# Convolution and two MLPs on one core: the taps' band by another way through DRAM, the first steps reordered

## The chip, the cores and the metric

The kernel runs on one core of one Trainium2 chip. Its time is the device time of one execution in microseconds, here the median of several runs. The engines are TensorE (PE, its weight loads shown as PEld), VectorE (DVE), ScalarE (ACT), GpSimd (POOL) and SyncE (SP), which here issues all DMAs, in program order. Each engine works through its own queue in order and waits on semaphores.

## What is computed

```python
# x: (2, 4096, 192), weight: (8 heads, 7 taps); 24 channels per head
w = weight - np.max(weight, axis=-1, keepdims=True)
w = np.exp(w)
w = w / (np.sum(w, axis=-1, keepdims=True) + 1e-09)
out = np.einsum('hk,bskhg->bshg', w, x_unf)   # causal convolution over 7 positions
...
h = x @ w_in1                                  # first MLP, 192 -> 2048 -> 192
x = np.maximum(0.01 * h, h) @ w_out1
...
h = x @ w_in2                                  # second MLP
P = a[0] + a[1] * h + a[2] * h2 + a[3] * h3
Q = 1.0 + np.abs(b[0]) * np.abs(h) + np.abs(b[1]) * h2
out = (P / (Q + 1e-06)) @ w_out2
```

## The kernel before

The 8192 tokens go through in 16 blocks of 512 (`COLS`). A block is convolved on TensorE (`convolve`, L673): per head, a 110 x 104 matrix of taps (`band`, each row the taps' row moved by one) is the weight, and five tiles of 104 tokens with 6 tokens of halo stream past. ScalarE and VectorE copy the result out of PSUM (`copy_conv`), TensorE transposes it (`transpose_x`, L687, L688), and ScalarE and VectorE split it (`split_xt`) into a high part and a low part, so that fp32r products keep fp32's accuracy. `xs[0]` holds three parts: high and low of the first 128 channels, and the stacked high and low of the last 64. The first MLP's input to the second is split the same way into `xs[1]` (`split_x2`).

The MLPs run in pairs of hidden tiles: 8 pairs per block (`STEPS`), 128 in all. For pair m, `up` (L713) makes ten passes, five for each half: parts 0, 0, 1, 2, 2 of `xs`. Then come the leaky ReLU, its high part and its low part (L447, L451, L601), and `down` (L723 to L733), ten passes. For the second MLP, the steps between `up` and `down` are |h|, the slope and the first power on ScalarE (L390, L398, L405), the denominator on POOL (L337), the reciprocal (L411, L414), and polynomial, quotient, product and residue on VectorE (L593, L595, L575, L581, L587). The second MLP's pair n runs in step n together with the first MLP's pair n + 10 (`LEAD`), so the steps begin at -10. A step's place in its block is its phase, n modulo 8. In phase 7 a block is convolved, in phase 6 transposed, in phase 7 the second MLP's input is split.

The order on each engine is written out by hand, in `step(n)` of that engine. TensorE does `up` of the second MLP, then convolution, transposes or output transposes if the phase has them, then `up` and `down` of the first MLP. Block 0 is convolved in front of step -10 and block 1 in step -4. Block 2 is convolved in step -1. Before the first convolution TensorE runs `WARM_UP` matmuls on the identity, once POOL has made it.

The start also loads the weights. The weights of both MLPs come in 16 pieces (`order`), staged in seven buffers (`stage_weights` on SP), and each is split into a high part on ScalarE (`split_hi`, L373) and a low part on VectorE (`split_lo`, L510 or L515 and L517). How many pieces are split behind each pair is the tuple `share` in `split_with`. A piece of `w_in` takes one operation on each engine; a piece of `w_out` one on ScalarE and two on VectorE.

The band is made thus: SP loads `weight` to all 128 partitions; VectorE and ScalarE make the softmax; POOL has zeroed two rows of 852 numbers on one partition (L328), into which VectorE writes the taps (L545); SP writes both rows to DRAM (L301), and reads them back to 110 partitions, each shifted by one element (L303), as 110 x 8 pieces of 104 numbers. `band` is laid out by head, so that the weight of head h, `band[:, h, :]`, is contiguous in each partition.

Of the kernel before, what the change touches and what calls it, by code (L numbers as in the profile page):

```python
# [27 lines left out]
P = 128  # L28
# [14 lines left out]
WARM_UP = 30  # L43


def conv_mlp_mlp(nc: bass.Bass, x, weight, w_in1, w_out1, w_in2, w_out2, a, b, out):
# [24 lines left out]
    with ExitStack() as ctx:  # L71
# [31 lines left out]
        band = sb("band", [CROWS, H, CT])  # L103
        taps = sb("taps", [P, H, K])
        tap_stat = sb("tap_stat", [P, 3, H])
# [3 lines left out]
        conv_row = conv_sb[:, :, :].rearrange("p a c -> p (a c)")  # L109
        out_row = out_cm[:, :, :].rearrange("p a c -> p (a c)")  # L110

        tap_rows = [t[0:1, 0:HEADS * ROW].rearrange("p (h j) -> p h j", h=HEADS) for t in (conv_row, out_row)]
        tap_dram = nc.dram_tensor("tap_rows", (H, ROW), F32, kind="Internal").ap()
# [30 lines left out]
        s_const = sem("consts_loaded")  # L144
# [5 lines left out]
        s_row = sem("tap_row_steps")  # L150
# [110 lines left out]
        def _(sp):  # L261
# [27 lines left out]
            sp.dma_start(taps[:, :, :], weight.partition_broadcast(P)).then_inc(s_const, 16)  # L289
            sp.dma_start(coef_a[:, :], a.partition_broadcast(P)).then_inc(s_const, 16)  # L290
            sp.dma_start(coef_b[:, :], b.partition_broadcast(P)).then_inc(s_const, 16)
            sp.wait_ge(s_zero, 1)
            load_x(0)

            stage_weights(0)
            stage_weights(1)
            sp.wait_ge(s_row, 4)
            for half, row in enumerate(tap_rows):  # L300
                sp.dma_start(tap_dram[half * HEADS:(half + 1) * HEADS, :], row).then_inc(s_row_out, 16)  # L301
            sp.wait_ge(s_row_out, 32)
            sp.dma_start(band[:, :, :], bass.AP(tap_dram.tensor, 0, [[1, CROWS], [ROW, H], [1, CT]])).then_inc(s_band, 16)  # L303
# [20 lines left out]
        def _(pool):  # L324
            nc.gpsimd.memset(zero_halo[:, :], 0.0).then_inc(s_zero, 1)
            nc.gpsimd.memset(eye[:, :], 0.0).then_inc(s_eye, 1)
            for row in tap_rows:
                nc.gpsimd.memset(row, 0.0).then_inc(s_row, 1)  # L328
# [32 lines left out]
        def _(act):  # L361
# [64 lines left out]
            def step(n):  # L426
# [11 lines left out]
                if n >= 0 and phase != CONV_AT:  # L438
                    slope(n)
                if runs(conv_block(n), BLOCKS):  # L440
                    copy_conv(conv_block(n))
                if n >= 0:
                    first_power(n)
                    if phase == CONV_AT:
                        slope(n)
# [54 lines left out]
        def _(dve):  # L500
# [25 lines left out]
            dve.wait_ge(s_const, 48)  # L526
            stat = [tap_stat[:, k, :] for k in range(3)]

            def over_taps(v):
                return v.unsqueeze(2).to_broadcast([P, H, K])  # L530
# [11 lines left out]
            dve.wait_ge(s_row, 2)  # L542
            for half, row in enumerate(tap_rows):
                heads = slice(half * HEADS, (half + 1) * HEADS)
                V.tensor_tensor(row[:, :, CT - 1:CT - 1 + K], taps[0:1, heads, :],  # L545
                                tap_stat[0:1, 2, heads].unsqueeze(2).to_broadcast([1, HEADS, K]),
                                ALU.mult).then_inc(s_row, 1)

            V.scalar_tensor_tensor(coef_b[:, :], coef_b[:, :], -1.0, coef_b[:, :],
                                   ALU.mult, ALU.max).then_inc(s_coef, 1)  # L550
# [105 lines left out]
            split_lo(0)  # L656
            split_lo(1)
            copy_conv(0)
# [3 lines left out]
            V.tensor_tensor(eye2[:, :], eye[:, 0:DR], eye[:, DR:P], ALU.add).then_inc(s_eye2, 1)  # L662
            every_step(step, tail)

        @block.tensor
        def _(pe):
            T = nc.tensor

            def convolve(c):

                pe.wait_ge(s_x, 16 * (CTILES + 1) * (c + 1))
                for h in range(H):
                    last = T.matmul(conv_ps(c, h // HEADS)[:, h % HEADS], band[:, h, :],  # L673
# [30 lines left out]
            def up(m, pair0, dst, rest_ready, done):  # L704

                for half in range(2):
# [3 lines left out]
                    for j, (lhs, part) in enumerate(terms):  # L710
                        if half == 0 and j == 3:
                            rest_ready()
# [23 lines left out]
            def step(n):  # L736
# [15 lines left out]
                if runs(n, PAIRS):  # L752
                    if phase == 0:
                        pe.wait_ge(s_x2_lo, 2 * (n // STEPS) + 1)
                    if n == 0:
                        pe.wait_ge(s_wlo, 2 * PIECES)
# [4 lines left out]
                    def x2_rest_ready():  # L761
                        if phase == 0:
                            pe.wait_ge(s_x2_lo, 2 * (n // STEPS) + 2)

                    up(1, n, hidden_2(n), x2_rest_ready, s_h2)


                if convolves:
# [25 lines left out]
                def up_1():  # L794
                    if runs(m0, PAIRS):
                        if m0 in (0, STEPS // 2):
                            pe.wait_ge(s_wlo, 2 if m0 == 0 else 5)
                        if transposes:
                            pe.wait_ge(s_xt_lo, 2 * (m0 // STEPS) + 1)

                        if convolves and conv_block(n) > 1:
                            pe.wait_ge(s_conv_a, conv_block(n) + 1)
                            pe.wait_ge(s_conv_b, conv_block(n) - 1)
                        if leaves:
# [3 lines left out]
                        def xt_rest_ready():  # L808
                            if transposes:
                                pe.wait_ge(s_xt_lo, 2 * (m0 // STEPS) + 2)  # L810

# [102 lines left out]
```

## Time and profile before

| | us |
|---|---|
| median of 3 runs | 1302.13 |
| lowest and highest | 1301.85, 1303.23 |
| the profiled execution | 1303.33 |
| its span, first to last instruction | 1300.7 |
| TensorE busy in the span | 1254.8 |
| VectorE, ScalarE, POOL busy | 1039.7, 1042.9, 611.3 |
| mean granted clock of TensorE | 0.987 |

Times in the trace count from the first instruction. The profiled execution is 2.6 us longer than its own span, which leaves out what lies around the program. A group of matmuls such as "x16" counts passes: an fp32 matmul is two passes, so the eight of a convolution are 16. The clock is given as a share of full speed, 2.4 GHz.

### The profile page before, as it was taken

What the parts mean: (1) busy time and instruction counts of PE and PEld (TensorE: products, weight loads), DVE (VectorE), ACT (ScalarE), POOL (GpSimd) and SP (SyncE); (2) the same over time, 40 slices, a digit from 0 to 9 for tenths busy, and PEclk for the clock granted to TensorE, in tenths of its full rate; (3) what the DMA queues carried; (4) which work ended last, traced back from release to release, by engine and by line L of the source; (5) the groups of instructions that cost most, each with busy time, mean ns of one, the idle gap of its engine ahead of it and who ended that gap; (6) DMA issues with size and microseconds to landing.
All of it is one profiled execution on the core that took longest, in us unless ns stands there. A gap on an engine that the chain in (4) does not pass through costs nothing.

```text
span 1300.7 us, 14911 instructions
## 1 busy us (share of the span) xinstructions
PE 1254.8 (96%) x5788; PEld 1034.8 (80%) x5788; DVE 1039.7 (80%) x901; ACT 1042.9 (80%) x1025; POOL 611.3 (47%) x264
## 2 busy tenths in 40 slices
PE   6979999999999999999999999999999999999866
PEld 5768888888888888888888888888888888878744
DVE  2648878888788888888888788878878788887886
ACT  3768888888888888888888888888888888888874
POOL 0014454545545455454454544545545445454563
PEclk8999999999999999999999999999999999999898
DMA  6300000000000000000000000000000000000000
GB/s 184 94 14 1 1 26 2 26 1 1 26 1 26 1 19 7 2 26 1 26 1 1 26 1 26 1 27 1 1 26 1 26 1 13 1 1 14 0 13 12
DMA packets 25092, 21.73 MB, mean 17 GB/s; under 512 B 2909, under 2 KB 23997, under 8 KB 25023
## 3 DMA queue, kind: packets, MB, share of 16 engines
q1 hardware_dynamic: 25023, 20.80, 5.5%
q8 instruction: 45, 0.74, 0.2%
q14 instruction: 24, 0.20, 0.0%
HBM read 14.49 MB, written 6.30 MB: 16 GB/s over the span
## 4 chain that ended last, share of the span: by engine, by line
PE 90%; POOL 3%; issue 3%; DVE 2%; ACT 2%; DMA 1%; POOLq 0%; SPq 0%; ACTq 0%; DVEq 0%
PE h L713 43%; PE acc L723 8%; PE acc L732 8%; PE acc L733 8%; PE acc L725 8%; PE acc L724 8%; PE h L673 2%; POOL lo L342 1%; POOL den L337 1%; PE h L700 1%; POOL pol L337 1%; PE h L699 1%; PE h L687 0%; PE h L688 0%; ACT hi L451 0%
## 5 line engine op out<-in xcount | busy, mean ns | idle before, releaser
L713 PE MATMUL h<-xs,wa 128*128 128x512 f32 x2530 | 608.8, 392 | 16.4 <-DVE den L587 4.8
L337 POOL TENSOR_TENSOR den<-den,rec 128x1024 f32<-128x1024 f32 x125 | 300.9, 2407 | 665.7 <-DVE den L587 415.5
L713 PEld LDWEIGHTS h<-xs,wa 128*128 128x128 f32 x2530 | 475.6, 189 | 124.5 <-issue 9.2
L342 POOL TENSOR_TENSOR lo<-den,rec 128x1024 fp32r<-128x1024 f32 x124 | 299.4, 2414 | 6.7 <-DVE den L587 6.7
L575 DVE SCALAR_TENSOR_TENSOR hi<-pol,coef_a,rec 128x1024 fp32r<-128x1024 f32 x118 | 151.6, 1285 | 109.8 <-issue 68.8
L732 PE MATMUL acc<-lo,wb 128*128 128x512 f32 x512 | 201.1, 393 | 8.5 <-POOL lo L342 8.5
L723 PE MATMUL acc<-hi,wb 128*128 128x512 f32 x512 | 204.7, 400 | 2.7 <-ACT out_cm L464 1.4
L390 ACT ACTIVATE rec<-h 128x1024 f32<-128x1024 f32 x125 | 128.4, 1027 | 97.4 <-PE h L713 90.6
L725 PE MATMUL acc<-hi,wb 128*128 128x512 f32 x512 | 200.8, 392 | 0.0
L724 PE MATMUL acc<-hi,wb 128*128 128x512 f32 x512 | 200.7, 392 | 0.0
L733 PE MATMUL acc<-lo,wb 128*128 128x512 f32 x512 | 200.4, 391 | 0.0
L593 DVE TENSOR_TENSOR pol<-pol,h 128x1024 f32<-128x1024 f32 x125 | 152.6, 1220 | 58.8 <-ACT pol L405 55.5
L601 DVE TENSOR_TENSOR lo<-h,hi 128x1024 fp32r<-128x1024 f32 x128 | 156.2, 1220 | 46.5 <-ACT hi L451 46.5
L447 ACT ACTIVATE h<-h 128x1024 f32<-128x1024 f32 x128 | 129.3, 1010 | 61.8 <-PE h L713 61.8
L411 ACT ACTIVATE rec<-den,one 128x1024 f32<-128x1024 f32 x125 | 143.8, 1150 | 35.1 <-POOL den L337 35.1
L398 ACT ACTIVATE den<-rec,coef_b 128x1024 f32<-128x1024 f32 x125 | 155.9, 1247 | 3.1
L581 DVE SCALAR_TENSOR_TENSOR den<-den,hi 128x1024 f32<-128x1024 f32 x125 | 154.2, 1234 | 4.3
L587 DVE SCALAR_TENSOR_TENSOR den<-pol,coef_a,den 128x1024 f32<-128x1024 f32 x118 | 151.6, 1285 | 4.1
L595 DVE SCALAR_TENSOR_TENSOR pol<-pol,coef_a,h 128x1024 f32<-128x1024 f32 x118 | 151.2, 1281 | 4.2
L405 ACT ACTIVATE pol<-h,coef_a 128x1024 f32<-128x1024 f32 x125 | 149.4, 1195 | 0.4
L414 ACT ACTIVATE rec<-rec 128x1024 f32<-128x1024 f32 x128 | 135.9, 1062 | 4.1
L451 ACT ACTIVATE hi<-h 128x1024 fp32r<-128x1024 f32 x128 | 131.6, 1028 | 8.5 <-PE acc L733 4.6
(105 smaller groups left out, 959.4 us busy)
## 6 DMA issues: line engine op xcount, KB each, us to landing
out<-out_tok SPq DMA_DIRECT2D x16, 384.0 KB, 2.8
x_tok<-in_x SPq DMA_DIRECT2D x64, 82.5 KB
rec<-in_moe_w_out SPq DMA_DIRECT2D x4, 384.0 KB, 4.4
x_tok<-in_x SPq DMA_DIRECT2D x16, 78.0 KB
pol<-in_moe_w_out SPq DMA_DIRECT2D x3, 384.0 KB, 4.0
pol<-in_moe_w_in SPq DMA_DIRECT2D x2, 512.0 KB, 6.2
den<-in_moe_w_in SPq DMA_DIRECT2D x2, 512.0 KB, 4.7
rec<-in_moe_w_in SPq DMA_DIRECT2D x4, 256.0 KB, 5.4
```

What stands on the lines that cost most here:

```text
L337: nc.gpsimd.tensor_tensor(den_of(n)[:, :], den_of(n)[:, :], rec[n % RECS][:, :], ALU.mult).then_inc(s_den, 1)
L342: nc.gpsimd.tensor_tensor(lo2[n % 2][:, :], den_of(n)[:, :], rec[n % RECS][:, :], ALU.mult).then_inc(s_lo2, 1)
L398: nc.scalar.activation(den_of(n)[:, :], rec[n % RECS][:, :], ACT.Identity, scale=coef_b[:, 1:2], bias=coef_b[:, 0:1]).then_inc(s_slope, 1)
L581: V.scalar_tensor_tensor(den_of(n)[:, :], den_of(n)[:, :], 1.000001, hi2[k][:, :].bitcast(F32), ALU.add, ALU.mult).then_inc(s_back, 1)
L593: V.tensor_tensor(pol_of(n)[:, :], pol_of(n)[:, :], hidden_2_all(n), ALU.mult).then_inc(s_pol2, 1)
L601: V.tensor_tensor(lo1[k][:, :], hidden_1_all(m - LEAD), hi1[k][:, :].bitcast(F32), ALU.subtract).then_inc(s_lo1, 1)
L713: last = T.matmul(dst[:, half, :], lhs, xs[m][:, part, :], start=(j == 0), stop=(j == 4))
L723: T.matmul(acc[m][:, 0, :], w_hi, hi[:, cols], start=first and half == 0, stop=False)
L724: T.matmul(acc[m][:, 0, :], w_lo, hi[:, cols], start=False, stop=False)
L725: T.matmul(acc[m][:, 1, :], w_mix, hi[:, cols], start=first and half == 0, stop=False)
L732: T.matmul(acc[m][:, 0, :], w_hi, lo[:, cols], start=False, stop=stop)
L733: last = T.matmul(acc[m][:, 1, :], w_mix, lo[:, cols], start=False, stop=stop)
```

## The change

- The band's way. `weight` goes to one partition only. The zeros beside the taps are written to DRAM from a small zeroed rectangle (`flank`, part of `out_cm`, 8 partitions x 2 x 103), before x is loaded. The softmax is done on one partition, and its 56 results go in one piece between those zeros. The row in DRAM now holds the heads innermost, so that each partition of the band is one contiguous run of 832 numbers. `band` has the shape rows x 104 x 8, and the weight of head h is `band[:, :, h]`, with eight elements (32 B) from one to the next.
- The order on SP and VectorE at the start. The taps' write goes ahead of weight piece 1, the coefficients `a` and `b` are loaded behind the band, and VectorE's first convolution copy goes ahead of its split of piece 1. POOL no longer zeroes two rows.
- `WARM_UP` is 28, not 30.
- The splits of the last two weight pieces move from step -3 to steps -2 and -1.
- In step -1, `up` goes ahead of the convolution of block 2, which goes to PSUM tensor `h1`; its copies on ScalarE go behind the leaky ReLU.
- In steps 0 and 1, ScalarE does the first power ahead of the slope.
- The waits of `up` for x: in blocks 0 and 1 the first pass waits for the high part alone, the third for the low part, the fourth for the rest. The second MLP's `up` waits likewise at each block's start, except in the tail, where it waits for all parts at once.

```diff
-WARM_UP = 30
+WARM_UP = 28
...
-        band = sb("band", [CROWS, H, CT])
-        taps = sb("taps", [P, H, K])
+        band = sb("band", [CROWS, CT, H])
+        taps = sb("taps", [1, H, K])
+        tap_kh = sb("tap_kh", [1, K, H])
+        flank = out_cm[0:H, :, 0:CT - 1]
...
-            share = (1, 2, 2, 2, 2, 2, 0, 2)
+            share = (1, 2, 2, 2, 2, 2, 0, 0, 1, 1)
...
+            sp.dma_start(taps[:, :, :], weight.partition_broadcast(1)).then_inc(s_taps, 16)
+            sp.wait_ge(s_flank, 1)
+            sp.dma_start(bass.AP(tap_dram.tensor, 0, [[CT - 1, H], [(CT - 1 + K) * H, 2], [1, CT - 1]]),
+                         flank).then_inc(s_row_out, 16)
+            sp.wait_ge(s_zero, 1)
+            load_x(0)
+            stage_weights(0)
+            sp.wait_ge(s_row, 1)
+            sp.dma_start(bass.AP(tap_dram.tensor, (CT - 1) * H, [[K * H, 1], [1, K * H]]),
+                         tap_kh[:, :, :].rearrange("p k h -> p (k h)")).then_inc(s_row_out, 16)
+            stage_weights(1)
+            sp.wait_ge(s_row_out, 32)
+            sp.dma_start(band[:, :, :].rearrange("p i h -> p (i h)"),
+                         bass.AP(tap_dram.tensor, 0, [[H, CROWS], [1, CT * H]])).then_inc(s_band, 16)
...
-                if n >= 0 and phase != CONV_AT:
+                if n >= 2 and phase != CONV_AT:
                     slope(n)
-                if runs(conv_block(n), BLOCKS):
+                if runs(conv_block(n), BLOCKS) and n != -1:
                     copy_conv(conv_block(n))
...
+                if n == -1:
+                    copy_conv(conv_block(n))
                 for j in range(*split_with(m0)):
                     split_hi(j)
...
             split_lo(0)
+            copy_conv(0)
             split_lo(1)
-            copy_conv(0)
...
-                    last = T.matmul(conv_ps(c, h // HEADS)[:, h % HEADS], band[:, h, :],
+                    last = T.matmul(conv_ps(c, h // HEADS)[:, h % HEADS], band[:, :, h],
...
+            def xt_ready(c, j):
+                if j == 0 and c < 2:
+                    pe.wait_ge(s_xt_hi, 2 * c + 1)
+                if j == (2 if c < 2 else 0):
+                    pe.wait_ge(s_xt_lo, 2 * c + 1)
+                if j == 3:
+                    pe.wait_ge(s_xt_hi, 2 * c + 2)
+                    pe.wait_ge(s_xt_lo, 2 * c + 2)
...
                 alone = n < -LAG2
                 catch_up = n == -LAG2
-                if convolves or transposes or leaves:
+                if n == -1:
+                    up_1()
+                    h1_free()
+                    convolve(conv_block(n))
+                elif convolves or transposes or leaves:
```

SP's queue at the program's start, before and then now. `taps`, `coef_a` and `coef_b` are the small inputs, `tap_rows` and `tap_row` the tensor in DRAM, `pol0` and `pol1` the staging buffers of weight pieces 0 and 1.

```order
L289 DMA taps<-in_weight 128x56
L290 DMA coef_a<-in_moe2_a 128x4
L291 DMA coef_b<-in_moe2_b 128x2
L267 DMA x_tok<-in_x 104x192
L267 DMA x_tok<-in_x 110x192 x4
L269 DMA x_tok<-zero_halo 6x192
L280 DMA pol0<-in_moe_w_in 128x1024
L282 DMA pol1<-in_moe_w_in 64x1024
L283 DMA pol1<-in_moe_w_in 64x1024
L301 DMA tap_rows<-conv_sb 1x852
L301 DMA tap_rows<-out_cm 1x852
L303 DMA band<-tap_rows 110x8x104
```

```order
L289 DMA taps<-in_weight 1x56
L291 DMA tap_row<-out_cm 8x2x103
L267 DMA x_tok<-in_x 104x192
L267 DMA x_tok<-in_x 110x192 x4
L269 DMA x_tok<-zero_halo 6x192
L280 DMA pol0<-in_moe_w_in 128x1024
L297 DMA tap_row<-tap_kh 1x56
L282 DMA pol1<-in_moe_w_in 64x1024
L283 DMA pol1<-in_moe_w_in 64x1024
L301 DMA band<-tap_row 110x832
L303 DMA coef_a<-in_moe2_a 128x4
L304 DMA coef_b<-in_moe2_b 128x2
```

The taps' write stands one weight piece further ahead, the band's read has only the two halves of piece 1 between itself and that write, and the coefficients stand behind the band.

VectorE's queue in steps -3 to -1, before and then now. `lo1_` is the leaky ReLU's low part, `wb1` the second MLP's output weights, `xs0` the split x, `fold` and `xs1` the second MLP's split input.

```order
L601 TENSOR_TENSOR lo1_1<-h2,hi1_1 128x1024
L515 TENSOR_TENSOR wb1<-pol0,wb1 128x4x64
L517 TENSOR_TENSOR wb1<-pol0,wb1 128x4x128
L515 TENSOR_TENSOR wb1<-pol1,wb1 128x4x64
L517 TENSOR_TENSOR wb1<-pol1,wb1 128x4x128
L554 TENSOR_TENSOR xs0<-acc1,xs0 128x512
L557 TENSOR_TENSOR xs0<-acc1,xs0 64x512
L601 TENSOR_TENSOR lo1_0<-h1,hi1_0 128x1024
L563 TENSOR_TENSOR fold<-acc0,xs1 64x512
L565 TENSOR_TENSOR xs1<-acc0,xs1 128x512
L568 TENSOR_TENSOR xs1<-acc0,fold 64x512
L601 TENSOR_TENSOR lo1_1<-h2,hi1_1 128x1024
```

```order
L596 TENSOR_TENSOR lo1_1<-h2,hi1_1 128x1024
L549 TENSOR_TENSOR xs0<-acc1,xs0 128x512
L552 TENSOR_TENSOR xs0<-acc1,xs0 64x512
L596 TENSOR_TENSOR lo1_0<-h1,hi1_0 128x1024
L517 TENSOR_TENSOR wb1<-pol0,wb1 128x4x64
L519 TENSOR_TENSOR wb1<-pol0,wb1 128x4x128
L558 TENSOR_TENSOR fold<-acc0,xs1 64x512
L560 TENSOR_TENSOR xs1<-acc0,xs1 128x512
L563 TENSOR_TENSOR xs1<-acc0,fold 64x512
L596 TENSOR_TENSOR lo1_1<-h2,hi1_1 128x1024
L517 TENSOR_TENSOR wb1<-pol1,wb1 128x4x64
L519 TENSOR_TENSOR wb1<-pol1,wb1 128x4x128
```

The four operations on `wb1` stood ahead of the split of x; now two stand behind the next pair's low part, and two behind the one after.

TensorE's queue at the border of steps -2 and -1, before and then now: the last passes of `down` of pair 7, then the convolution of block 2 and the `up` of pair 9, then `down` of pair 8.

```order
L732 MATMUL acc0<-lo1_1,wb0 128x512
L733 MATMUL acc0<-lo1_1,wb0 128x512
L673 MATMUL h1<-x_tok,band 104x120 x8
L713 MATMUL h2<-xs0,wa0 128x512 x10
L723 MATMUL acc0<-hi1_0,wb0 128x512
L724 MATMUL acc0<-hi1_0,wb0 128x512
```

```order
L748 MATMUL acc0<-lo1_1,wb0 128x512
L749 MATMUL acc0<-lo1_1,wb0 128x512
L729 MATMUL h2<-xs0,wa0 128x512 x10
L671 MATMUL h1<-x_tok,band 104x120 x8
L739 MATMUL acc0<-hi1_0,wb0 128x512
L740 MATMUL acc0<-hi1_0,wb0 128x512
```

`up` and the convolution have changed places.

## Rows read from the trace of the kernel before

**Rows 1.** The page, part 1: TensorE's busy time, share of the span, instructions.

```profile
PE 1254.8 (96%) x5788; PEld 1034.8 (80%) x5788; DVE 1039.7 (80%) x901; ACT 1042.9 (80%) x1025; POOL 611.3 (47%) x264
```

**Rows 2.** Busy time by stretch (us): stretch, length, each engine's busy time, TensorE's clock, DMA.

```profile
50.00:75.00 25.00, 21.01 (x109) 16.97 (x108) 12.58 (x18) 13.01 (x17) 0.00 (x0) 1.00 0.09 25
...
175.00:1200.00 1025.00, 1023.32 (x4767) 848.29 (x4766) 848.90 (x720) 856.39 (x839) 510.48 (x214) 1.00 0.04 11
```

**Rows 3.** Timeline, first 10 us: start, length, engine, line, operation, idle before it.

```profile
1.83 0.80 POOL L328 MEMSET out_cm<- 1x852 f32 x1
...
2.15 1.99 SPq L267 DMA_DIRECT2D x_tok<-in_x  x5
...
3.01 8.62 PE L891 MATMUL h<-eye 128*128 128x128 f32 x60 [3.01 <-POOL eye L330]
...
9.69 1.06 ACT L373 ACTIVATE wa<-pol 128x1024 fp32r<-128x1024 f32 x1 [2.61 <-DMA pol<-in_moe_w_in]
```

**Rows 4.** The chain that ended last, in order of time: start, length, what.

```profile
7.29 4.12 DMA tap_rows<-out_cm
...
11.44 4.46 DMA band<-tap_rows
...
15.94 2.80 PE acc L673 x16
...
21.57 0.60 ACT xs L489
...
23.04 4.38 PE h L713 x10
...
27.44 1.02 ACT h L447
...
35.65 2.27 PE h L713 x10
```

**Rows 5.** Busy time by stretch, first 31 us; the granted clock stands before the DMA share.

```profile
16.80:23.00 6.20, 3.89 (x20) 3.29 (x19) 1.43 (x3) 1.95 (x4) 0.00 (x0) 0.50 0.73 192
...
26.90:30.80 3.90, 2.79 (x12) 1.90 (x11) 1.26 (x2) 3.33 (x4) 0.00 (x0) 0.99 0.85 219
```

**Rows 6.** Timeline, 62 to 84 us: VectorE and TensorE.

```profile
62.65 0.68 DVE L517 TENSOR_TENSOR wb<-pol,wb 128x512 fp32r<-128x512 f32 x1
...
64.19 0.68 DVE L554 TENSOR_TENSOR xs<-acc,xs 128x512 fp32r<-128x512 f32 x1
...
64.92 2.62 PE L713 MATMUL h<-xs,wa 128*128 128x512 f32 x10 [1.69 <-DVE xs L554]
...
70.95 1.89 PE L673 MATMUL h<-x_tok,band 110*104 110x120 f32 x16 [1.14 <-DVE lo L601]
...
74.01 2.55 PE L713 MATMUL h<-xs,wa 128*128 128x512 f32 x10 [1.17 <-ACT conv_sb L377]
...
80.06 4.12 PE L713 MATMUL h<-xs,wa 128*128 128x512 f32 x17 [1.24 <-DVE lo L601]
```

**Rows 7.** Timeline, 83 to 130 us: the passes of steps 1 and 2.

```profile
88.74 4.83 PE L713 MATMUL h<-xs,wa 128*128 128x512 f32 x20 [1.61 <-DVE pol L595]
...
97.37 4.83 PE L713 MATMUL h<-xs,wa 128*128 128x512 f32 x20 [1.53 <-DVE pol L595]
```

**Rows 8.** Instructions of one line: duration ns min/median/max, first and last start, forms.

```profile
L673 PEld LDWEIGHTS h<-x_tok,band x224: 166/170/171, 71.0 to 1068.5; 110*104 110x104 f32 x112
...
L673 PE MATMUL h<-x_tok,band x224: 263/266/350, 71.0 to 1068.6; 110*104 110x120 f32 x112
...
L687 PEld LDWEIGHTS h<-eye,conv_sb x70: 138/141/143, 135.8 to 1134.4; 104*128 104x128 f32 x70
...
L891 PEld LDWEIGHTS h<-eye x60: 192/192/338, 3.0 to 11.2; 128*128 128x128 f32 x60
```

**Rows 9.** Timeline, the tail: x2's last split and the pass that reads it.

```profile
1218.12 0.69 DVE L568 TENSOR_TENSOR xs<-acc,fold 64x512 fp32r<-64x512 f32 x1
...
1219.54 2.43 PE L713 MATMUL acc<-xs,wa 128*128 128x512 f32 x10
```

More of the change, by code:

```diff
@@ L108, in conv_mlp_mlp @@
         one = sb("one", [P, 1])
[L109 to L113, printed above, removed]
+        flank = out_cm[0:H, :, 0:CT - 1]
+        tap_dram = nc.dram_tensor("tap_row", (ROW * H,), F32, kind="Internal").ap()
         stage = [t[:, :] for t in (*pol, *den, *rec)]
@@ L297, in _ @@
             stage_weights(0)
+            sp.wait_ge(s_row, 1)
+            sp.dma_start(bass.AP(tap_dram.tensor, (CT - 1) * H, [[K * H, 1], [1, K * H]]),
+                         tap_kh[:, :, :].rearrange("p k h -> p (k h)")).then_inc(s_row_out, 16)
             stage_weights(1)
-            sp.wait_ge(s_row, 4)
-            for half, row in enumerate(tap_rows):
-                sp.dma_start(tap_dram[half * HEADS:(half + 1) * HEADS, :], row).then_inc(s_row_out, 16)
             sp.wait_ge(s_row_out, 32)
-            sp.dma_start(band[:, :, :], bass.AP(tap_dram.tensor, 0, [[1, CROWS], [ROW, H], [1, CT]])).then_inc(s_band, 16)
+            sp.dma_start(band[:, :, :].rearrange("p i h -> p (i h)"),
+                         bass.AP(tap_dram.tensor, 0, [[H, CROWS], [1, CT * H]])).then_inc(s_band, 16)
+            sp.dma_start(coef_a[:, :], a.partition_broadcast(P)).then_inc(s_const, 16)
+            sp.dma_start(coef_b[:, :], b.partition_broadcast(P)).then_inc(s_const, 16)
             for k in range(2, 5):
@@ L324, in _ @@
         def _(pool):
+            nc.gpsimd.memset(flank, 0.0).then_inc(s_flank, 1)
             nc.gpsimd.memset(zero_halo[:, :], 0.0).then_inc(s_zero, 1)
             nc.gpsimd.memset(eye[:, :], 0.0).then_inc(s_eye, 1)
-            for row in tap_rows:
-                nc.gpsimd.memset(row, 0.0).then_inc(s_row, 1)
             pool.wait_ge(s_eye, 1)
@@ L541, in _ @@
             dve.wait_ge(s_tap, 6)
[L542 to L550, printed above, removed]
+            V.tensor_tensor(tap_kh[:, :, :].rearrange("p k h -> p h k"), taps[:, :, :], over_taps(stat[2]),
+                            ALU.mult).then_inc(s_row, 1)
             def split_xt(c):
@@ L702, in transpose_out, with x2_ready, up @@
                 last.then_inc(s_ot, 1)
-            def up(m, pair0, dst, rest_ready, done):
+            def xt_ready(c, j):
[6 more added lines that the diff above has]
+                    pe.wait_ge(s_xt_lo, 2 * c + 2)
+            def x2_ready(n, j):
+                c = n // STEPS
+                if n % STEPS == 0 and j == 0:
+                    pe.wait_ge(s_x2_hi, c + 1)
+                if n % STEPS == 0 and j == 2:
+                    pe.wait_ge(s_x2_lo, 2 * c + 1)
+                if n % STEPS == 0 and j == 3:
+                    pe.wait_ge(s_x2_lo, 2 * c + 2)
+            def up(m, pair0, dst, ready, done):
                 for half in range(2):
@@ L710, in up @@
                     for j, (lhs, part) in enumerate(terms):
-                        if half == 0 and j == 3:
-                            rest_ready()
+                        if half == 0:
+                            ready(j)
                         last = T.matmul(dst[:, half, :], lhs, xs[m][:, part, :], start=(j == 0), stop=(j == 4))
@@ L759, in step @@
                         pe.wait_ge(s_lo1, LEAD)
[L761 to L768, printed above, removed]
+                    up(1, n, hidden_2(n), lambda j: x2_ready(n, j), s_h2)
+                if convolves and n != -1:
                     if conv_block(n) > 1:
@@ L797, in up_1 @@
                             pe.wait_ge(s_wlo, 2 if m0 == 0 else 5)
-                        if transposes:
-                            pe.wait_ge(s_xt_lo, 2 * (m0 // STEPS) + 1)
-                        if convolves and conv_block(n) > 1:
+                        if convolves and conv_block(n) > 1 and n != -1:
                             pe.wait_ge(s_conv_a, conv_block(n) + 1)
                             pe.wait_ge(s_conv_b, conv_block(n) - 1)
+                        if n == 0:
+                            pe.wait_ge(s_conv_a, 3)
+                            pe.wait_ge(s_conv_b, 1)
                         if leaves:
@@ L806, in up_1 @@
                         hidden_1_free()
[L808 to L812 removed]
+                        up(0, m0, hidden_1(n), lambda j: xt_ready(m0 // STEPS, j) if transposes else None, s_h1)
                 def down_1(lag):
```

34 lines of the change are left out of this document (15 added, 19 removed).

## The prediction, made before the changed kernel ran

> **What bounds the kernel now.** I read three views in this order. The page gives TensorE 1254.8 of 1300.7 us busy [rows 1]. The busy time by stretch says where the missing 46 us are: between 175 and 1200 us TensorE idles 1.7 of 1025 us, while 50 to 75 us alone lacks 4.0 us [rows 2]. So nothing is to be won in the middle except by less TensorE work, and every microsecond that the start is shortened by shifts all that follows. The last view is the chain of waits through the first 90 us, where each link that the change touches is to be found.
>
> The start is a serial chain [rows 4]: the taps' rows go to DRAM (issued 7.29, landed 11.41), the band is read back (4.46 us, landed 15.90), eight convolution matmuls (16 passes) follow, then copies and transposes until 21.57, then the split of x, and the first ten passes of `up` run from 23.04 to 27.44, where the first leaky ReLU begins. From there the order of pairs is fixed and soon bound by TensorE. The granted clock is half (1.2 GHz) from 16.8 to 26.9 us [rows 5], after 4.3 us of an idle TensorE between the warm-up's end at 11.63 [rows 3] and the band.
>
> **The band earlier (part of the front).** Before, the rows' writes are issued behind the first two weight pieces. Now only the 8 x 2 x 103 zeros go early (after a POOL memset of a few tenths at 0.75), and the 56 taps go between piece 0 and piece 1. SP issues taps, flank, x (1.99 us, with the halo 2.8) and piece 0 [rows 3]; without the two coefficient DMAs and with the flank it is some 0.5 us ahead of before. ScalarE could use piece 0 at 9.69 [rows 3]; that becomes about 9.2, and the taps' write, queued right behind it, lands with it at 9.2, not 11.41. The softmax of the taps is off the path: it waits for 56 numbers on one partition and no longer for the coefficients, so it ends before SP has issued piece 0. The band is then issued at 9.2. At its old price (4.46 us) it lands at 13.7; below, 3.0 us (12.2), since it is 110 runs of 3,328 B and not 880 of 416 B, but piece 1 is still ahead of it in the queues. Nearest to the old row and somewhat below it I take 3.6: the band lands at **12.8**, 3.1 us earlier. The Trainium skill (DMA: Bandwidth & Descriptors, Specifications) wants at least 512 B per transfer for line rate, which speaks for the shorter end.
>
> **From the band to the first leaky ReLU** it is 27.44 - 15.94 = 11.50 us now [rows 4]. If the clock stays full: the convolution takes 1.89 instead of 2.80 (rows 6 have it at full clock), -0.9; the ten transposes likewise, -0.9. From the copy of the transposed x at 21.57 to 27.44 it is 5.87 now. The first pass now waits only for the high half (0.60 after it), but the fourth still needs the second low half, 2.05 us after the copy's start (0.6 + 0.7 + 0.7); then seven passes at 0.227 and the latency, 1.8. That is 3.85, -2.0. Together **-3.8**. If the clock still falls, only the earlier first passes count: 2.05 + 7 x 0.43 + 0.2 = 5.25, -0.6. For a full clock speaks that the two row memsets (0.80 each, rows 3) no longer precede the identity, so the warm-up begins near 1.9 and not 3.01, and with 28 for 30 matmuls ends near 10.0 to 10.8; the idle gap is 2 to 2.8 us, not 4.3. Against it, convolution and transposes are sparse work with two gaps of 0.8 us. VectorE's split of piece 1 now stands behind its convolution copy; `up` waits for it, but it runs (1.2 us) under the transposes.
>
> **Steps -2 to 0 (the middle).** TensorE's last pass ends at 63.23 (64.92 less 1.69 of idling, rows 6); the next could start 0.15 earlier, at 63.08, but waits till 64.92 for the low half of x, because VectorE does two weight pieces first (the first ends at 63.33, the second as long again) and ScalarE two before its copy [rows 6]. With both moved away, ScalarE copies at 61.1 and 61.7 and VectorE subtracts at 62.3 and 63.0, ready at 63.7; the new per-part waits let `up` start at 63.08 with the fourth pass at 63.77: no wait left. Next, the convolution waited for the leaky ReLU (70.95, 1.14 idle), and `up` for the convolution's copies (74.01, 1.17), and step 0 for the next leaky ReLU (80.06, 1.24) [rows 6]. With `up` ahead of the third convolution these become back to back work: three units of ten passes, 2.27 each [rows 4] (up, down, up) from 63.08 to 69.9, convolution 1.64 to 71.5, down 2.27. One new wait: that down needs the x2 split, which stands on VectorE behind the leaky's low part (68.9) and one weight piece (0.95): 69.8 + 3 x 0.7 = 71.95, so 0.4 us. It ends at 74.25; the leaky's low part of pair 9 is done at 73.4, the last weight piece at 75.0, before |h| can begin at 76.7. So step 0 begins at 74.25 and not 80.06: **-5.8**. This is queue order and holds whatever the front does.
>
> **First powers before slopes (n < 2).** The polynomial of pair 0 gets its first power 1.15 us sooner, so the wait of 1.61 at 88.74 [rows 7] falls to 0.5. But the slope, and with it POOL's denominator, moves back: pair 0's residue ends 0.7 us later after |h| than now. The polynomial of pair 1 stands on VectorE behind that residue, and the `up` of step 2, which needs it, now begins 17.31 us after that of step 0 (80.06 in rows 6 to 97.37 in rows 7); by the new queue 17.3. The second wait grows from 1.5 to 2.6: sum **0**. The polynomial of pair 2 waits for its own first power, not for the residue, so nothing is left of it from step 3 on.
>
> **The rest.** x2's wait split by part in each block: TensorE does not wait there now [rows 2]. In the tail the whole x2 is waited for at once; VectorE ends it at 1218.81, and TensorE comes to that pass at 1219.54 without a wait [rows 9]: 0, with 0.7 us of cover. Coefficients are needed near 76 us: 0. The added queue entries on SP (128-row coefficient DMAs ahead of piece 2) have some 4 us of slack before ScalarE reaches piece 2.
>
> **The band's layout on TensorE.** `band[:, :, h]` is now read with 32 B between elements, in 256 weight loads; no load here is strided. Now a band load takes 170 ns, and passes follow each other about every 103 ns ((1.89 - 0.35)/15, rows 6, 8). From 128 columns (192 ns, warm-up) and 104 (170) [rows 8] a column costs 0.92 ns, a load some 96 ns of its own time, hidden with 7 ns to spare. The lower end is 0; the upper a column at twice the price: 191 - 103 = 88 ns per load, in 15 blocks x 16 = 240 loads on the path 21 us. I take 0, because the transposes load 128 columns in 141 ns [rows 8]: the port gives a contiguous column in clearly less time than the band's load uses, so there is slack for a slower read.
>
> **Sum.** -3.1 - 3.8 - 5.8 + 0 = -12.7 on a span of 1300.7, which is 1288.0. The profiled run was 1303.33, 2.6 above its span, the median of three 1302.13, 1.4 above it; so **1289.4**.
>
> **Rivals.**
> (a) The clock falls all the same: -3.1 - 0.6 - 5.8 = -9.5, 1292.6. Rows 5 show it falling 5.2 us after the warm-up, so a fall at about 15 would still be possible.
> (b) The band stays bound to piece 1 in the queues and lands near 14.9, with the clock down: -1.0 - 0.6 - 5.8 = -7.4, 1294.7. For it: DMA is busy throughout. The same place is reached with a strided load that sticks out by 25 ns (240 x 25 ns = 6 us, 1295.4). A part of this case, with 45 ns, ends within 0.2% of before.
> (c) Slower: the strided load takes twice its time per column. Place: the 15 convolutions on the path. 1289.4 + 21 = 1310.5. It decides from 12.7/240 = 53 ns per load on, a load 1.6 times as long as now. Against it are the transposes' loads; for it, that the slack is 7 ns only. The Trainium skill (SBUF — State Buffer, the note on cachelines) says that reads that go to a new 16-byte line with every access pay a penalty, and gives none in ns; 32 B between elements is such a read. By that rule the change would end slower; no run here shows it yet.
>
> **How the numbers follow.** Forecast (full clock) 0.48, (a) 0.27, (b) 0.10 of which 0.02 lies within 0.2%, (c) 0.15. Two tenths of a per cent, 2.6 us, is about what a measurement of this kernel can tell from no change. Faster: 0.83; same: 0.02; slower 0.15. The low end is the forecast with the band at 12.2 (-0.6), without the new wait of 0.4, and less the scatter of the three runs of before (1301.85 to 1303.23, 1.4): 1287.0; the high end takes in (a), (b) with its two halves together (1294.7 + 6), 1300.7. Left out are (c) and a few per cent at the ends.
>
> **What would show it.** Band landed (first convolution pass) at 12.2 to 13.7; granted clock 1.0 up to 25 us, or half again; the first leaky ReLU at 20.5 (full) or 23.8; no wait before `up` of step -2; 10.8 to 11.3 us from there to the `up` of step 0 (15.1 now); waits of 0.5 and 2.6 in steps 1 and 2; band loads still near 170 ns and sixteen passes in 1.9 us. I am wrong if the latter take 2.5 us or more, or if the first up of the second product doesn't come 12 to 13 us earlier than 80.06.

## The result, and the profile of the changed kernel

| | before | changed |
|---|---|---|
| median of the runs (4 and 4, same chip), us | 1302.42 | 1313.49 |
| lowest and highest | 1301.85, 1303.23 | 1311.78, 1314.01 |
| the profiled execution | 1303.33 | 1311.78 |
| its span | 1300.7 | 1310.0 |
| TensorE busy | 1254.8 | 1271.1 |

The ratio is 1.0082, with a 95% interval of 1.0065 to 1.01: the change makes the kernel slower by 0.8%. The prediction was 1289.4, faster. What happened is its rival (c).

The first look goes to what TensorE is busy with. The page's part 1 (against [rows 1]):

```profile
PE 1271.1 (97%) x5784; PEld 1055.6 (81%) x5784; DVE 1038.6 (79%) x900; ACT 1044.5 (80%) x1025; POOL 609.8 (47%) x263
```

TensorE is 16.3 us busier, with the same passes but for the four that the warm-up has fewer, and its weight loads 20.8 us; no other engine changed by more than 2. So some pass has become dearer. The instructions of the convolution's line and of the transposes' (duration min/median/max; against [rows 8]):

```profile
L671 PEld LDWEIGHTS h<-x_tok,band x224: 267/290/292, 70.1 to 1078.7; 110*104 110x104 f32 x112
L671 PE MATMUL h<-x_tok,band x224: 266/357/358, 70.3 to 1078.8; 110*104 110x120 f32 x112
...
L685 PEld LDWEIGHTS h<-eye,conv_sb x70: 138/140/142, 131.1 to 1144.5; 104*128 104x128 f32 x70
```

The load of the band takes 290 ns and not 170; the transposes' load, whose source did not change, is where it was. What that makes of a convolution shows the chain that ended last, in the steady state, first before and then after (start, length, what):

```profile
146.25 1.64 PE h L673 x16
```

```profile
141.50 3.01 PE h L671 x16
```

Sixteen passes take 3.01 us instead of 1.64, 86 ns more for each pass: I read it so that the load no longer hides behind the pass ahead of it and sets the pace (3.01/16 = 188 ns). The load's own record grew by more, 120 ns; how much of a record is reading and how much waiting, the profile does not show. These two lines hold the second half of the story as well: at this place the changed kernel is 4.75 us ahead. The front and the middle did gain; the convolutions then eat the gain and more.

The chain through the first 80 us of the changed kernel, against [rows 4]:

```profile
4.82 3.96 DMA tap_row<-tap_kh
8.79 5.51 DMA band<-tap_row
14.35 3.56 PE acc L671 x16
...
21.48 4.76 PE h L729 x10
26.26 1.02 ACT h L447
...
48.06 3.01 PE acc L671 x16
...
63.42 2.47 PE h L729 x10
...
70.44 3.01 PE h L671 x16
...
75.78 2.28 PE h L729 x10
```

The first leaky ReLU begins at 26.26 (27.44 before), the second convolution at 48.06 (49.26 before), the first `up` of the second MLP at 75.78 (80.06 before). In the changed kernel's stretches (stretch, length, busy time of each engine, granted clock, DMA share, GB/s) one sees that the middle is now dense and that the clock fell all the same; against [rows 2, 5]:

```profile
16.80:23.00 6.20, 4.58 (x20) 3.35 (x18) 3.32 (x5) 2.60 (x4) 0.00 (x0) 0.50 0.66 168
...
50.00:75.00 25.00, 25.00 (x120) 21.17 (x120) 12.06 (x17) 13.59 (x17) 0.00 (x0) 1.00 0.08 21
```

TensorE has no idle time left between 50 and 75 us. What it waits for in the first 140 us (total, times, longest):

```profile
PE acc L671 <- DMA band<-tap_row: 4.2, 1, 4.2
PE h L729 <- DVE pol L590: 3.0, 2, 2.6
...
PE h L729 <- DVE lo L596: 1.1, 1, 1.1
...
PE h L729 <- ACT xs L491: 0.8, 1, 0.8
```

**The account.** By the chain, a convolution of the changed kernel begins earlier by 1.2 us in block 1 and by 4.75 in block 3, and later by 8.96 in block 15:

```profile
1067.18 1.64 PE h L673 x16
```

```profile
1076.14 3.01 PE h L671 x16
```

So each of the twelve blocks between loses (4.75 + 8.96)/12 = 1.14 us: 1.37 more in its convolution, less 0.23 given back elsewhere. The chain shows where: the twenty passes of `up` after a convolution, first before, then after:

```profile
231.52 4.82 PE h L713 x20
```

```profile
229.22 4.53 PE h L729 x20
```

The end of VectorE's polynomial, which these passes need, again before and after:

```profile
230.09 1.28 DVE L595 SCALAR_TENSOR_TENSOR pol<-pol,coef_a,h 128x1024 f32<-128x1024 f32 x1
```

```profile
226.46 1.28 DVE L590 SCALAR_TENSOR_TENSOR pol<-pol,coef_a,h 128x1024 f32<-128x1024 f32 x1
```

In the kernel before it ends at 231.37, 0.15 us ahead of the passes, so they had just waited for it. Now it ends at 227.74, 1.5 us ahead, and 0.3 us of the convolution's loss are hidden. The experiments below bear this out: in both kernels these twenty passes take 4.53 us in the steady blocks when the loads are dear, and 4.70 to 4.82 when they are not. That the wait for the polynomial is the link is argued from the times.

### The profile page after: what moved, and what is told of

The parts are those of the page before. It is cut to its first block, busy times and chain, and to the rows that moved or that the text cites. A ratio compares the mean times of both kernels' runs of the same rounds, so it can differ in the third digit from the quotient of the medians.

```text
span 1310.0 us, 14916 instructions
## 1 busy us (share of the span) xinstructions
PE 1271.1 (97%) x5784; PEld 1055.6 (81%) x5784; DVE 1038.6 (79%) x900; ACT 1044.5 (80%) x1025; POOL 609.8 (47%) x263
## 4 chain that ended last, share of the span: by engine, by line
PE 90%; POOL 3%; issue 2%; DVE 2%; ACT 1%; DMA 1%; SPq 0%; POOLq 0%; ACTq 0%; DVEq 0%
PE h L729 42%; PE acc L739 8%; PE acc L748 8%; PE acc L749 8%; PE acc L741 8%; PE acc L740 8%; PE h L671 3%; POOL lo L342 1%; POOL den L337 1%; PE h L698 1%; PE h L697 1%; POOL pol L337 1%; PE acc L671 1%; PE h L685 0%; PE h L686 0%
```

## The experiments

All times are medians; the kernel before lay at 1302.3 to 1302.8 on the chips of the experiments.

**The layout undone.** The changed kernel with the band by head again, in DRAM and on the core, and so with its read in 880 runs of 416 B again. Everything else is kept:

```diff
-band = sb("band", [CROWS, CT, H])
+band = sb("band", [CROWS, H, CT])
-sp.dma_start(band[:, :, :].rearrange("p i h -> p (i h)"),
-             bass.AP(tap_dram.tensor, 0, [[H, CROWS], [1, CT * H]]))
+sp.dma_start(band[:, :, :], bass.AP(tap_dram.tensor, 0, [[1, CROWS], [ROW, H], [1, CT]]))
...
-band[:, :, h],
+band[:, h, :],
```

> The changed kernel with the band's old layout alone put back (row in DRAM by head, band read as 110 x 8 pieces of 104, weight loads contiguous); all else as changed. Theory L (the strided weight load costs the time: sixteen passes of a convolution 3.01 us against 1.64): 15 blocks x 1.37 = 20.6 us less, and 0.8 in the first convolution: 1313.5 - 21.4 = about 1292, loads back at 170 ns. Rival R (the loss lies in the front's DMA queue or in the waits by part): stays above 1305. Of the band's own read: if its 5.51 us (4.46 before) come from the pieces of 3,328 B it falls to about 4.5; if from piece 1 and the coefficients around it, it stays at 5 or more.

Measured: 1292.66 (1288.46 to 1294.23), ratio 0.9921 [0.9899, 0.9944].

```profile
L670 PEld LDWEIGHTS h<-x_tok,band x224: 167/170/171, 67.3 to 1060.9; 110*104 110x104 f32 x112
```

One change of order in the band turns 0.8% slower into 0.8% faster. The rest of the edit is worth 9.6 us against the kernel before on the same chip, and the layout costs 20.8. Not all of the 20.8 is in the loads: in the profile of this run the band also landed 1.4 us earlier (12.89 and not 14.30). Between the convolutions of blocks 3 and 15, where nothing else differs, the layout costs 1.22 us per block.

**One-piece band, but contiguous loads.** The band lands as in the changed kernel, in a buffer that is free at that time, and VectorE copies it once, by head; only the first convolution reads it strided.

```diff
+V.tensor_copy(band2[:, :, :, :], band[:, :, :].rearrange("p i (q s) -> p q i s", s=STR)).then_inc(s_band2, 1)
...
-band[:, :, h],
+band[:, :, h] if c == 0 else band2[:, h // STR, :, h % STR],
```

> The changed kernel, where VectorE copies the band once into the old layout after it has landed; only the first convolution reads with 32 B between elements (in the buffer out_cm, which is free then), all others read contiguously. Theory L: 15 x 1.37 = 20.6 us less than the changed kernel, about 1293; the copy (832 elements, about 1 us) lies under the first convolution. The front stays as it is (band landed at 14.35). Rival R: above 1305.

Measured: 1294.14 (1291.15 to 1294.78), ratio 0.9933 [0.9915, 0.9951]. The copy took 0.92 us, under other work. It cures the loss as well as the old layout; the one-piece read has no gain to show for it.

**The kernel before with the strided layout alone.** A copy turns the landed band into the layout of the change, for blocks 1 to 15.

```diff
+V.tensor_copy(band2[:, :, :].rearrange("p i h -> p h i"), band[:, :, :]).then_inc(s_band2, 1)
...
-band[:, h, :],
+band[:, h, :] if c == 0 else band2[:, :, h],
```

> The kernel before, in which only the layout of the weight loads is changed: VectorE copies the landed band into the layout with 32 B between elements, which blocks 1 to 15 use. Theory L: 1302.4 + 15 x 1.37 = 1323, loads of 290 ns. If the price per block is only the 1.15 us by which the distance between convolutions grew in the changed kernel, 1319.7, and the other 0.2 us are no gain of the other edits. Rival R: within 3 us of 1302.

Measured: 1321.69 (1321.21 to 1322.67), ratio 1.015 [1.0135, 1.0165].

```profile
L679 PEld LDWEIGHTS h<-x_tok,band x224: 267/291/292, 73.1 to 1089.1; 110*104 110x104 f32 x112
```

The layout alone costs the kernel before 19.4 us, of which 1.13 in each block of the steady state. In the profile of this run the clock also fell from 76 to 83 us, and ten passes of `up` there took 4.62 us and not 2.56, so some 2 us of this run are not the loads' own. Removing the layout and adding it move the time by about the same, in the steady blocks by 1.22 and 1.13 us each: this cause is shown.

**How the price goes with the stride.** The run with the copy, its elements 8 B and 16 B apart instead of side by side:

```diff
-STR = 1
+STR = 2    # the other run: 4
```

> As e2_copy with two heads innermost: 8 B between elements, two elements per 16-byte piece. Theory P: two reads per line hide the price, the load stays at 170 ns and the time at e2_copy's 1294. Rival Q (any distance costs, in proportion): a load of about 185 to 200 ns, which sticks out of the 103 ns slot: 1296 to 1300.

> As e2_copy, but the copy's layout has four heads innermost: 16 B between the elements of a weight load, one element per 16-byte piece. Theory P (a price for each new 16-byte line, as the Trainium skill's note on cachelines says; measured here 290 against 170 ns at 32 B): the load is as dear as at 32 B, 290 ns, a convolution 3.0 us, the time some 17 us over e2_copy's 1294.1. Rival Q (the price grows with the distance): a load of about 230 ns.

Measured: 8 B apart 1296.41 (1293.3 to 1296.73), 0.9949 [0.9933, 0.9966]; 16 B apart 1311.16 (two runs, 1310.21 and 1312.1), 1.007 [1.005, 1.009]. The loads, first 8 B, then 16 B:

```profile
L678 PEld LDWEIGHTS h<-x_tok,band x224: 172/174/175, 67.7 to 1061.4; 110*104 110x104 f32 x112
```

```profile
L678 PEld LDWEIGHTS h<-x_tok,band x224: 264/287/288, 68.7 to 1076.3; 110*104 110x104 f32 x112
```

170, 174, 287, 290 ns for 4, 8, 16 and 32 B between elements: not a price per byte, but a step between 8 and 16 B, and 32 B costs no more than 16. That is what the Trainium skill (SBUF — State Buffer, the note on cachelines) says of 16-byte lines, here for TensorE's weight loads. With two elements to a line the load is 4 ns longer, but a convolution still takes 1.64 us, and from block 3 to block 15 it is 920.1 us as with the contiguous copy; the 2.3 us between the two medians lie elsewhere, in the profiles at the front and in the clock. The runs show the step; that lines of 16 B are what makes it is the explanation of the Trainium skill, which no run here tests apart. The note's sentence that one can stride 4 fp32 for free fits only if it counts the elements of a line: a stride of 4 fp32 is the 16 B here, and costs 117 ns a load.

**The middle alone.** The kernel before with the weights' splits moved and the third convolution behind `up`:

```diff
-share = (1, 2, 2, 2, 2, 2, 0, 2)
+share = (1, 2, 2, 2, 2, 2, 0, 0, 1, 1)
+if n == -1:
+    up_1()
+    h1_free()
+    convolve(conv_block(n))
...
```

> The kernel before with the middle alone: last two weight splits moved to steps -2 and -1, up ahead of the third convolution in step -1; waits for x as before. Theory M (my sum of the middle): step 0's up 5.0 to 5.8 us earlier (the wait for both low parts of x stays late by some tenths without the waits by part), 1302.4 - 5.5 = about 1297. Rival: VectorE's later splits are handed on to steps 0 and 1, and less than 3 us are left: above 1299.4.

Measured: 1296.92 (1294.09 to 1298.72), ratio 0.9958 [0.9944, 0.9971], 5.3 us less than before. The chain has `up` of step -2 and of step 0 at

```profile
62.84 2.42 PE h L715 x10
74.35 2.28 PE h L715 x10
```

11.5 us apart (15.1 in [rows 6], where 1.69 of waiting stood ahead of it besides). One short new wait lies between, for x2's split:

```profile
71.76 0.50 PE L725 MATMUL acc<-hi,wb 128*128 128x512 f32 x1 [0.33 <-DVE xs L570]
```

**The order of powers and slopes undone**, in the run with the copy:

```diff
-if n >= 2 and phase != CONV_AT:
+if n >= 0 and phase != CONV_AT:
     slope(n)
...
-    if phase == CONV_AT or n < 2:
+    if phase == CONV_AT:
         slope(n)
```

> e2_copy with the slope ahead of the first power again in steps 0 and 1. My working: the two waits of TensorE before the up of steps 1 and 2 go from 0.4 and 2.6 to 1.6 and 1.4, their sum and the time stay within 0.5 us of e2_copy. Rival: the earlier first power was worth a microsecond: 1 us slower.

Measured: 1293.88 (1292.19 to 1294.16), 0.3 us from the run with the copy. The waits of steps 1 and 2 are back at their size of [rows 7]:

```profile
79.91 4.87 PE L736 MATMUL h<-xs,wa 128*128 128x512 f32 x20 [1.61 <-DVE pol L593]
...
88.57 4.83 PE L736 MATMUL h<-xs,wa 128*128 128x512 f32 x20 [1.53 <-DVE pol L593]
```

3.1 in two waits against 3.0 in the changed kernel: this part moves a wait and removes next to none.

**The waits by part undone**, in the run with the copy (the first pass again waits for the low part of the first 128 channels, of x and of x2, which the third needs):

```diff
-if j == 0 and c < 2:
-    pe.wait_ge(s_xt_hi, 2 * c + 1)
-if j == (2 if c < 2 else 0):
+if j == 0:
     pe.wait_ge(s_xt_lo, 2 * c + 1)
... (x2 likewise)
```

> The run with the contiguous copy of the band, and in it one edit undone: the first passes wait again for the whole of x's high terms and of x2, not for a part of each. The prediction priced these waits by part at 0 outside the middle. Theory A (they are worth something after all): in the profiles of the two kernels with the contiguous band, blocks 3 to 15 each run 0.07 us quicker than in the kernel before, in the kernel with the middle alone they do not; so this run loses 13 times 0.07, 0.9 us, and in the middle the 0.4 us between the wait for x2 by part and as a whole: about 1295.4 against 1294.1, and the start of block 15 less that of block 3 grows by 0.85 us against the run with the copy. Rival B (the 0.07 comes from elsewhere): that difference stays within 0.2 us.

Measured: 1297.2 (1296.19 to 1297.87), ratio 0.9955 [0.9938, 0.9971], 3 us above the run with the copy. Theory A falls: from block 3 to block 15 the two differ by 0.02 us, not 0.85. The 3 us are not all the edit's either. In this profile the band landed 1.4 us later, the clock was at half for 14 us at the front and not for 3, and it fell a second time. Its waits give the edit's own part:

```profile
PE h L732 <- DVE xs L552: 1.5, 1, 1.5
```

against 0.8 for ScalarE's part in the changed kernel: 0.7 us, once, at the front, and nothing where TensorE is full. Whether the longer wait also makes the lower clock more frequent is not shown. That the steady blocks run 0.07 us quicker than before in every version with the new front, and not in the one with the middle alone, stays unexplained. Part of it shows where the kernel waits for the polynomial: the twenty passes there take 4.70 to 4.78 us in the run with the layout undone, against 4.77 to 4.82 before.

**A longer warm-up**, the run with the copy and `WARM_UP = 40` instead of 28, to close the gap before the band:

> e2_copy with 40 warm-up matmuls, not 28: TensorE is busy until about 12.6 us, when the band lands (12.81 in e2_copy), and not until 10.2. Theory C (the idle stretch before the band is what makes the clock fall): the granted clock stays full through the first convolution, the first leaky ReLU starts at 19.5 to 20.5, and the median is 2 to 3 us under e2_copy's 1294.1. Rival: sparse work after it (the convolution with its two gaps) makes it fall all the same: within 1 us of e2_copy.

Measured: 1293.66 (1290.58 to 1295.15), 0.9932 [0.9911, 0.9953]. TensorE now waits 0.2 us for the band:

```profile
1.92 11.24 PE L904 MATMUL h<-eye 128*128 128x128 f32 x80 [1.92 <-POOL eye L333]
13.37 3.36 PE L678 MATMUL acc<-x_tok,out_cm 110*104 110x120 f32 x16 [0.21 <-DMA out_cm<-tap_row]
```

The convolution and the transposes ran at full clock, but the clock fell afterwards, and once more in step 2; stretches 12 to 16, 16 to 20, 20 to 24 and 86 to 92 us:

```profile
12.00:16.00 4.00, 3.79 (x25) 3.60 (x23) 1.17 (x2) 1.06 (x1) 0.00 (x0) 1.00 1.09 284
16.00:20.00 4.00, 2.38 (x16) 1.75 (x15) 2.47 (x3) 1.83 (x4) 0.00 (x0) 0.99 0.54 123
20.00:24.00 4.00, 3.98 (x11) 2.81 (x11) 1.94 (x6) 0.89 (x2) 0.00 (x0) 0.59 0.80 228
...
86.00:92.00 6.00, 3.86 (x10) 3.10 (x11) 4.63 (x5) 2.98 (x3) 4.49 (x2) 0.72 0.00 0
```

TensorE has only 2.38 of 4 us of work between 16 and 20; the fall moved behind this stretch, to the passes of `up`. No gain came of it.

**The band's read ahead of piece 1 of the weights**, and **the coefficients' transfers behind pieces 2 to 4**, each in the run with the copy:

```diff
-stage_weights(1)
 sp.wait_ge(s_row_out, 32)
 sp.dma_start(band ...)
+stage_weights(1)
```

> The run with the contiguous copy of the band, with the one change that SyncE issues piece 1 of the weights behind the band's read instead of ahead of it. The band landed at 12.8 to 14.4 us in every profile with the new front, whether its read was issued at 7.8 or at 8.8. Theory A (the read shares the engines with piece 1 and piece 2 and ends when they let it): without piece 1 in front of it, it ends near 12, 0.8 us or more before the 12.81 of the run with the copy. Rival B (its duration is its own): it still takes 4.3 to 5.6 us from its issue and lands at 12.8 or later. The splits of piece 1 come later, under the idle time of step -2's start, so the time stays within 1 us of 1294.1 if the band isn't earlier.

> The run with the contiguous copy of the band, with the two small coefficient transfers (partition broadcasts of a and b) issued behind pieces 2 to 4 of the weights instead of right behind the band's read. In the packets of the changed kernel's trace the coefficients' small packets lie at 11.4 to 13.8 us, among the band's last ones, which land at 13.7. Theory A (the coefficients hold up the band's last packets): the band lands 0.5 us or more earlier than the 12.81 of the run with the copy, the read takes under 3.8 us. Rival B: it takes 4.3 to 5.6 us as in the other runs.

Measured: band first 1292.78 (two runs), ratio 0.9923 [0.9903, 0.9943]; coefficients late 1295.68 (two runs), 0.9946 [0.9926, 0.9965]. Against the copy's 1294.14 neither is told apart by so few runs, but the chain is clear. First the run with the copy, then band first, then coefficients late:

```profile
8.54 4.27 DMA out_cm<-tap_row
```

```profile
7.66 4.41 DMA out_cm<-tap_row
```

```profile
7.85 6.63 DMA out_cm<-tap_row
```

Band first lands at 12.07, the earliest of these three, as theory A has it; but it does so by beginning 0.9 us earlier, ahead of piece 1 on SP's queue, and the read itself takes 4.41 us, as rival B has it. The coefficients are not what holds up the band: with them gone from behind it, it took 6.63. But pieces 2 to 4 then stood right behind it, and whether they slow it is not shown. In the profiles behind piece 1 the one-piece read takes 4.27 to 6.63 us (eight profiles), and the read in 880 runs 4.13 to 4.47 (four): the long runs did not shorten the read and seem to lengthen it.

**All together.** The old layout, the band's read first, `WARM_UP = 36`:

> The changed kernel with the old layout back (row in DRAM by head, band as 8 rows of 104 in each partition, so every convolution's weight load is contiguous and no copy is needed), with the band's read issued ahead of piece 1 of the weights, and with 36 warm-up matmuls in place of 28. Theory: as in the run with the band's read first, the band lands near 12.1 us, in 880 runs of 416 bytes as well as in 110 of 3,328; the warm-up then ends near 12.2 and TensorE hardly waits for the band; loads take 170 ns. In the profile of the changed kernel with the old layout the middle and the steady state were right, so the time is that of the run with the band first less what the clock gives back: 1291 us, 1288.5 to 1293. Rivals: with the old layout the read behind no piece of weights is slower than the one-piece read and lands at 12.9 or later, then 1292 to 1293.5; or the granted clock falls right behind the warm-up's end as in the run with 40, then as the run with the band first, 1292.8.

Measured: 1293.32 (1290.99 to 1293.61), ratio 0.9919 [0.9906, 0.9933], 2.3 us above the 1291 expected. It is faster than both kernels, but no faster than the version with only the old layout (1292.66). The band was no longer what ended last:

```profile
8.04 0.31 SPq L300 DMA_DIRECT2D band<-tap_row  x1
11.68 1.86 PE L670 MATMUL acc<-x_tok,band 110*104 110x120 f32 x16
```

Issued at 8.04 and there by 11.68, this read took 3.6 us at most, in 880 runs of 416 B and with no piece of weights ahead of it, against 4.41 for the 110 long runs in the same place. The convolution ran at full clock right behind the warm-up. Then the next link turned up in the chain:

```profile
9.02 4.96 DMA pol<-in_moe_w_in
...
14.00 1.06 ACT wa L372
15.06 0.47 ACT conv_sb L376
```

ScalarE takes its queue in order: its part of the convolution's copy stands behind its split of piece 1 of the weights, and piece 1, now issued behind the band, landed at 13.98 only. TensorE waited 2.0 us there:

```profile
PE acc L684 <- ACT conv_sb L376: 2.0, 1, 2.0
```

So the wait moved from the band to the piece that had been put behind it. Behind this wait the clock fell too (0.50 from 16 to 20 us), and again in step 2 (0.72 from 86 to 92).

## Why the prediction was wrong, step by step

- **The band's layout: the step that failed.** "I take 0, because the transposes load 128 columns in 141 ns." The load went from 170 to 290 ns, the pass from 103 to 188. The argument measured how fast a contiguous column comes, and this says nothing of a strided one. The working had the right end beside it: an upper bound of 88 ns per load, 21 us, with 86 ns measured, and a cover of 7 ns, too thin for a price of 0 to be likely. Both numbers, and the rule of the Trainium skill beside (c), pointed the other way; the chance of 0.15 for (c) was the misjudgement, and left the result outside the range. (c) gave 1310.5, and the run 1313.49: the 0.23 us given back in each of 13 blocks take 3.0 from it, and the front, which (c) took from the forecast, adds 5.8 (the next two points), which comes to 1313.3. The mechanism of (c), twice the time per column, gave 191 ns for the load; the measured pace is 188.
- **The band at 12.8: missed in the changed kernel (14.3).** The taps' write was in time: it landed at 8.79, before the 9.2 forecast. But the read took 5.51 us and not 3.6. Behind piece 1 it never took less than 4.27 in 110 runs of 3,328 B, and never less than 4.13 in 880 of 416 B, and the one read of 3.6 or less was of short runs. "Somewhat below the old row" was wrong; the old row's 4.46 would have been the better term. What the Trainium skill (DMA: Bandwidth & Descriptors, Specifications) asks for, transfers of at least 512 B, spoke for the shorter end; for this read the runs do not bear it out.
- **From the band to the leaky ReLU, -3.8 at full clock: missed.** The clock fell, at 12.4 us. 14.35 to 26.26 is 11.9 us, 0.4 more than before, where the forecast had 7.7 and rival (a) 10.9. The fall came before the convolution, so all of it ran at half clock (3.56 us; with the old layout 3.54, so at half clock the strided loads cost this one nothing). The idle gap was 4.2 us, as long as before: the warm-up ended earlier by as much as the band came. Even where the gap was closed, the clock fell in this stretch.
- **Steps -2 to 0, -5.8: right.** Alone, the middle gave 5.3 us. In the changed kernel 12.36 us lie between the two `up`, of which 1.37 is the dearer convolution; 11.0 against 11.2 forecast. The new wait of 0.4 for x2 was 0.33 in the run with the middle alone; in the changed kernel the longer convolution covers it.
- **First powers, 0: right.** Waits of 0.33 and 2.6 against forecasts of 0.5 and 2.6; undone, 0.3 us.
- **x2's waits by part, 0: right** where TensorE is full; at the front the waits by part of x are worth 0.7 us. **Tail, 0:** the pass that reads x2 still begins 0.7 us behind it.

Without the layout, the changed kernel comes to 1292.66: the case that the prediction had called (a), 1292.6. So the rest of the sum was sound in the main, with the clock's fall as the likelier case in place of the full clock. That the two numbers meet so closely is luck. In this run's profile the taps' write landed at 8.40 and not 9.2, and the band's read took 4.47 us and not 3.6, which together gave 12.89. From there to the leaky ReLU it took 11.9 us and not 10.9, and the steady blocks, priced at 0, gave back 0.9.

## What to carry to other kernels

A layout that suits a transfer must be priced at its readers first. Here one transfer of 4 us was reshaped, without being shortened, and 240 reads paid 86 ns each. If a load hides behind its pass with 7 ns to spare, an unmeasured access pattern is no term of 0: it is the first thing to measure. And a copy of 0.92 us under other work gives the readers their own layout where transfer and reader disagree.

## What was not expected of the hardware

- TensorE's load of 104 fp32 columns on 110 rows: 170 ns contiguous, 174 with 8 B between elements, 287 with 16 B, 290 with 32 B. Sixteen passes take 1.64 us with loads of 170 or 174 ns and 2.97 to 3.01 with loads of 287 or 290. At half clock the layout costs the passes next to nothing (3.56 against 3.54 us); the same strided convolution at full clock takes 3.37 (the run with `WARM_UP = 40`), the contiguous one 1.86 (all together).
- The band's read in one piece behind piece 1 took from 4.27 to 6.63 us, in programs that differ little or not at all up to there; in runs an eighth as long it took 4.13 to 4.47.
- The granted clock fell to half at some point between 12 and 20 us in every profile, and stayed there for 3 us in one and for 14 in another, though the programs are the same up to there; from the band to the leaky ReLU it took 9.6 us in the run with the copy and 11.8 in the one with 8 B, so some 2 us of scatter come from this alone. In five profiles it fell again between 86 and 98 us, behind the wait of 2.6 us in step 2. Such a second fall costs 1.6 us: the twenty passes there take 6.45 us instead of the 4.83 of [rows 7].

```profile
91.06 6.45 PE L732 MATMUL h<-xs,wa 128*128 128x512 f32 x20 [2.64 <-DVE pol L593]
```

The line is from the run with the waits undone. The reordered powers made waits of 0.3 and 2.6 us out of two of 1.6 and 1.5. With the 2.6, five of ten profiles have the second fall; with the old order, none of four has it there, though one of them (the kernel before with the strided layout) has a fall from 76 to 83 us. And the medians with and without the reordering, 1294.14 and 1293.88, show no loss. That is a weak hint and not a test.
